# The experts' first products with both halves of the rows in one 512-column matmul, and two changes at the seams

## The reference

```python
# attention: B, H, S, D = 2, 8, 768, 64; a state per head decays by lam
intra = einsum('bhic,bhjc->bhij', qb, kb) * Dmask
out   = einsum('bhij,bhjd->bhid', intra, vb) + (qb * lam_pow) @ kv_state
kv_state = lam_block * kv_state + (kb * rev_pow)^T @ vb

# MLP: 1536 rows, 512 -> 1536 -> 512
x = (silu(x @ w_gate) * (x @ w_val)) @ w_out

# experts: E = 8, F = 1024
expert_idx = argmax(x @ w_gate, axis=1)         # one expert per row
gate_w     = softmax value of the chosen expert
for e in range(E):
    xe = x[expert_idx == e]
    out[expert_idx == e] = gate_w * (maximum(xe @ w1[e], 0.0) @ w2[e])
```

## Time and profile before

| | |
|---|---|
| median of 3 runs | 570.27 us (569.58 to 571.07) |
| profiled execution | 570.9 us, its span 569.3 us |
| busy, share of the span | PE 96%, PEld 82%, DVE 57%, ACT 40%, POOL 14% |
| attention | 0 to 51 us |
| MLP and router | 51 to 361 us |
| index list, first gather | 361 to 374 us |
| experts | 374 to 569 us |

### The profile page before, as it was taken

The page is one execution under the profiler, slowest core; times in us unless marked ns, Lnnn a source line. Parts: engine busy times, 40 slices in busy tenths (PEclk is TensorE's granted clock), DMA queues, the critical chain, the costliest instruction groups (busy, mean ns, idle before and its releaser), DMA issues. The chain is left out here.

```text
span 569.3 us, 8791 instructions
## 1 busy us (share of the span) xinstructions
PE 549.3 (96%) x3290; PEld 468.1 (82%) x3290; DVE 322.4 (57%) x540; ACT 228.9 (40%) x369; POOL 78.6 (14%) x95
## 2 busy tenths in 40 slices
PE   6999999999999999999999999789999999999993
PEld 6888888888878888887888887579999999999982
DVE  8877545444655544545556665446666665766620
ACT  2115323332443432335434553245555554655510
POOL 6972000000000000000000010211130321311101
PEclk9999999999999999999999999979999999999998
DMA  8986433233213243223244545235565757554000
GB/s 295 300 277 209 163 111 107 64 108 111 99 69 122 82 149 111 74 92 111 62 141 151 170 161 221 94 117 209 220 239 181 269 180 246 205 189 164 20 8 34
DMA packets 18432, 84.45 MB, mean 148 GB/s; under 512 B 3036, under 2 KB 3036, under 8 KB 14816
## 3 DMA queue, kind: packets, MB, share of 16 engines
q1 hardware_dynamic: 13536, 71.35, 36.9%
q0 software_dynamic: 3712, 10.54, 5.4%
q10 hardware_dynamic: 1152, 2.13, 1.0%
HBM read 78.73 MB, written 7.39 MB: 151 GB/s over the span
## 5 line engine op out<-in xcount | busy, mean ns | idle before, releaser
L969 DVE TENSOR_TENSOR ewl<-stage,ewh 128x1024 fp32r<-128x1024 f32 x64 | 78.1, 1224 | 23.2 <-ACT ewh L813 23.2
L1090 DVE TENSOR_TENSOR sig<-bank,sig 128x512 f32<-128x512 f32 x36 | 24.9, 692 | 99.0 <-ACT sig L853 99.0
L608 PE MATMUL bank<-xh,gvh 128*128 (+1 forms) x288 | 77.1, 389 | 0.0
L608 PE MATMUL bank<-xl,gvh 128*128 (+1 forms) x288 | 77.0, 389 | 0.0
L608 PE MATMUL bank<-xh,gvl 128*128 (+1 forms) x288 | 77.0, 389 | 0.0
L813 ACT ACTIVATE ewh<-stage 128x1024 fp32r<-128x1024 f32 x64 | 67.0, 1052 | 0.9 <-DMA stage<-expert_w 0.9
L853 ACT ACTIVATE sig<-bank 128x512 f32<-128x512 f32 x36 | 21.7, 602 | 104.4 <-PE bank L608 104.4
L608 PEld LDWEIGHTS bank<-xl,gvh 128*128 128x128 f32 x288 | 54.1, 188 | 11.3
L608 PEld LDWEIGHTS bank<-xh,gvl 128*128 128x128 f32 x288 | 54.1, 188 | 11.2
L608 PEld LDWEIGHTS bank<-xh,gvh 128*128 128x128 f32 x288 | 54.0, 188 | 11.3 <-issue 0.2
L618 PE MATMUL bank<-hh,woh 128*128 128x512 f32 x144 | 56.8, 395 | 0.0
(11 more groups left out here) (144 smaller groups left out, 849.4 us busy)
## 6 DMA issues: line engine op xcount, KB each, us to landing
stage<-expert_w SPq DMA_DIRECT2D x28, 1024.0 KB, 4.9
stage<-mlp_w SPq DMA_DIRECT2D x36, 768.0 KB, 4.4
stage<-attn_in SPq DMA_DIRECT2D x24, 512.0 KB, 5.0
stage<-expert_w POOLq DMA_DIRECT2D x8, 512.0 KB, 5.6
x_rows<-x ACTq DMA_DIRECT2D x8, 260.0 KB, 5.1
x_rows<-x SPq DMA_DIRECT2D x4, 260.0 KB, 4.2
gx<-x_rows,idx POOLq DMA_INDIRECT x16, 4.5
out<-ys,idx POOLq DMA_INDIRECT x16, 3.9
```

The source lines that it names most:

```text
L608: last = mm(bank[:, where, :], wt[:, k, :], (xh, xl)[x][:, k, bass.ds(g * GT, GT)], start=(at == 0), stop=(at == 3 * KD - 1))
L969: V.tensor_tensor(dst, src, high.bitcast(F32), ALU.subtract).then_inc(inc, 1)
L1090: V.tensor_tensor(sig[:, :], bank[:, GATE_BANK, :], sig[:, :], ALU.mult).then_inc(sg_ready, 1)
```

## The change

**First products.** The tiles `exh` and `exl` become one tile `ex` with the high half at z = 0 and the low half at z = 1. `hidden` multiplies the high weights with both halves in one matmul of 512 columns, so that the left half of the PSUM bank gets high by high and the right half high by low; then the low weights with the high rows are added into the left half. The bank's halves have to be added afterwards: ACT copies the right one to `hx` (SBUF), DVE adds the left one to it and writes `hs`, ACT takes the relu of `hs`, and DVE the low half of it. PE's wait for a free bank is now on that addition.

**Rows of the next expert.** Their split and the exponents, all in slot 5 before, are spread over the slots 5, 6 and 7.

**Start.** ACT scales the keys of tile 0 (8 activations of 64 columns), POOL those of the other tiles and not before both decay tables are done; PE does the scores of tile 1 before the first product to the state.

**Before the experts.** POOL reads the number of rounds behind the first two gathers, not ahead of them.

```diff
-        exh = [sb(f"exh{i}", [P, KD, CAP], F32R, region2) for i in range(2)]
-        exl = [sb(f"exl{i}", [P, KD, CAP], F32R, region2) for i in range(2)]
+        ex = [sb(f"ex{i}", [P, 2, KD, CAP], F32R, region2) for i in range(2)]
+        hx = [sb(f"hx{i}", [P, CAP], F32, region2) for i in range(2)]
+        hs = [sb(f"hs{i}", [P, CAP], F32, region2) for i in range(2)]
...
             def keys(n):
                 s = n % 4
                 pool.wait_ge(kv_landed[s], n // 4 * 16 + 16)
-                pool.wait_ge(key_ready, 1)
+                pool.wait_ge(tables_ready, 2)
...
-            for n in range(NT):
+            for n in range(1, NT):
                 if n < LAST_STATE:
                     keys(n)
...
                 gather(0)
                 nc.gpsimd.memset(idx_now[0][:, :], 0).then_inc(now_ready, 2 * E)
                 gather(1)
+                n = read_passes(pool)
...
-            n = read_passes(pool)
-            first_pass()
+            n = first_pass()
...
-                pe.wait_ge(kd_ready, n + 1)
+                if n == 0:
+                    pe.wait_ge(first_keys, H)
+                else:
+                    pe.wait_ge(kd_ready, n)
...
             scores(0)
+            scores(1)
             to_state(0)
-            scores(1)
...
             def hidden(x, par, f):
                 pe.wait_ge(ewl_ready, x * NF2 + f + 1)
                 if f >= 2:
-                    pe.wait_ge(ehl_ready, x * NF2 + f - 1)
-                at = 0
-                for w, z in split_terms:
-                    for k in range(KD):
-                        last = mm(bank[:, H_BANK + f % 2, 0:CAP],
-                                  expert_bufs(par)[w][:, f, k * P:(k + 1) * P], (exh, exl)[z][par][:, k, :],
-                                  start=(at == 0), stop=(at == 3 * KD - 1))
-                        at += 1
+                    pe.wait_ge(hs_ready, x * NF2 + f - 1)
+                where = H_BANK + f % 2
+                for k in range(KD):
+                    mm(bank[:, where, :].rearrange("p (z c) -> p z c", z=2),
+                       expert_bufs(par)[0][:, f, k * P:(k + 1) * P], ex[par][:, :, k, :],
+                       start=(k == 0), stop=False, skip_group_check=True)
+                for k in range(KD):
+                    last = mm(bank[:, where, 0:CAP], expert_bufs(par)[1][:, f, k * P:(k + 1) * P],
+                              ex[par][:, 0, k, :], start=False, stop=(k == KD - 1), skip_group_check=True)
                 last.then_inc(eh_psum, 1)
...
+            act.wait_ge(kv_landed[0], 16)
+            act.wait_ge(key_ready, 1)
+            for h in range(H):
+                nc.scalar.activation(kd[0][:, h, :], att_part(0, 2)[:, h * D:(h + 1) * D], ACT.Copy,
+                                     scale=key_decay[:, h, :]).then_inc(first_keys, 1)
...
             def expert(x, par, more):
                 for f in range(NF2):
                     act.wait_ge(eh_psum, x * NF2 + f + 1)
-                    nc.scalar.activation(ehh[f % 2][:, :], bank[:, H_BANK + f % 2, 0:CAP],
-                                         ACT.Relu).then_inc(ehh_ready, 1)
+                    copy(hx[f % 2][:, :], bank[:, H_BANK + f % 2, CAP:]).then_inc(hx_ready, 1)
+                    act.wait_ge(hs_ready, x * NF2 + f + 1)
+                    nc.scalar.activation(ehh[f % 2][:, :], hs[f % 2][:, :], ACT.Relu).then_inc(ehh_ready, 1)
                     if more:
                         split_expert(1 - par, f, f // 2, expert_loads(x + 1, f // 2))
-                        if f == 5:
-                            tokens(x + 1, 1 - par)
+                        if f >= 5:
+                            (rows_high, rows_high, exponents)[f - 5](x + 1, 1 - par, f - 5)
...
+            def add_terms(x, f):
+                dve.wait_ge(hx_ready, x * NF2 + f + 1)
+                V.tensor_tensor(hs[f % 2][:, :], bank[:, H_BANK + f % 2, 0:CAP], hx[f % 2][:, :],
+                                ALU.add).then_inc(hs_ready, 1)
+
             def expert(x, par, more):
                 for f in range(NF2):
+                    add_terms(x, f)
                     dve.wait_ge(ehh_ready, x * NF2 + f + 1)
-                    V.scalar_tensor_tensor(out=ehl[f % 2][:, :], in0=bank[:, H_BANK + f % 2, 0:CAP], scalar=0.0,
+                    V.scalar_tensor_tensor(out=ehl[f % 2][:, :], in0=hs[f % 2][:, :], scalar=0.0,
                                            in1=ehh[f % 2][:, :].bitcast(F32), op0=ALU.max,
                                            op1=ALU.subtract).then_inc(ehl_ready, 1)
                     if more:
                         split_expert(1 - par, x + 1, f, f // 2)
-                        if f == 5:
-                            tokens(x + 1, 1 - par)
+                        if f >= 5:
+                            (rows_low, rows_low, gates)[f - 5](x + 1, 1 - par, f - 5)
```

More of the change, by code:

```diff
@@ L183, in bass_linear_attention_mlp_moe @@
         qs_ready = sem("qs_ready")
+        first_keys = sem("first_keys")
         kd_ready = sem("kd_ready")
@@ L240, in bass_linear_attention_mlp_moe @@
         eh_psum = sem("eh_psum")
+        hx_ready = sem("hx_ready")
+        hs_ready = sem("hs_ready")
         ehh_ready = sem("ehh_ready")
@@ L472, in first_pass @@
                     scatter(x)
+                return n
             def gather_by_copy(x, par):
@@ L904, in _, with rows_high, exponents @@
                 rows_out(NG - 1, t, t)
[L905 to L909, removed]
+            def rows_high(x, par, i):
+                act.wait_ge(gx_read, x * 2 + i + 3)
+                copy(ex[par][:, 0, :, i * P:(i + 1) * P],
+                     bank[:, T_BANK + i, :].rearrange("p (k i) -> p k i", k=KD)).then_inc(exh_ready, 1)
+            def exponents(x, par, i):
                 act.wait_ge(den_step, x * 2)
@@ L914, in tokens, with first_tokens @@
                 last.then_inc(expo_ready, 1)
+            def first_tokens(x, par):
+                for i in range(2):
+                    rows_high(x, par, i)
+                exponents(x, par, 2)
             def expert(x, par, more):
@@ L933, in last_expert @@
                     act.wait_ge(eh_psum, x * NF2 + f + 1)
-                    nc.scalar.activation(last_hidden(f, 0), bank[:, H_BANK + f % 2, 0:CAP],
-                                         ACT.Relu).then_inc(ehh_ready, 1)
+                    copy(hx[f % 2][:, :], bank[:, H_BANK + f % 2, CAP:]).then_inc(hx_ready, 1)
+                    act.wait_ge(hs_ready, x * NF2 + f + 1)
+                    nc.scalar.activation(last_hidden(f, 0), hs[f % 2][:, :], ACT.Relu).then_inc(ehh_ready, 1)
                 act.wait_ge(y_psum, x * 2 + 1)
@@ L949, in experts @@
                         split_expert(0, f, f // 2, expert_loads(base, f // 2))
-                tokens(base, 0)
+                first_tokens(base, 0)
                 with act.Fori(0, E // 2 - 1) as i:
@@ L1219, in _, with rows_low, gates @@
             V.tensor_scalar(passes[:, :], mosti[:, :], 8, None, ALU.logical_shift_right).then_inc(slots_ready, 1)
-            def tokens(x, par):
-                for i in range(2):
-                    low(exl[par][:, :, i * P:(i + 1) * P], bank[:, T_BANK + i, :].rearrange("p (k i) -> p k i", k=KD),
-                        exh[par][:, :, i * P:(i + 1) * P], exh_ready, x * 2 + i + 1, exl_ready)
+            def rows_low(x, par, i):
+                low(ex[par][:, 1, :, i * P:(i + 1) * P], bank[:, T_BANK + i, :].rearrange("p (k i) -> p k i", k=KD),
+                    ex[par][:, 0, :, i * P:(i + 1) * P], exh_ready, x * 2 + i + 1, exl_ready)
+            def gates(x, par, i):
                 dve.wait_ge(expo_ready, x + 1)
@@ L1230, in tokens, with first_tokens @@
                 V.reciprocal(gate_now[par][:, :], den_eps[:, :]).then_inc(gate_ready_x, 1)
+            def first_tokens(x, par):
+                for i in range(2):
+                    rows_low(x, par, i)
+                gates(x, par, 2)
+            def add_terms(x, f):
+                dve.wait_ge(hx_ready, x * NF2 + f + 1)
+                V.tensor_tensor(hs[f % 2][:, :], bank[:, H_BANK + f % 2, 0:CAP], hx[f % 2][:, :],
+                                ALU.add).then_inc(hs_ready, 1)
             def expert(x, par, more):
                 for f in range(NF2):
+                    add_terms(x, f)
                     dve.wait_ge(ehh_ready, x * NF2 + f + 1)
-                    V.scalar_tensor_tensor(out=ehl[f % 2][:, :], in0=bank[:, H_BANK + f % 2, 0:CAP], scalar=0.0,
+                    V.scalar_tensor_tensor(out=ehl[f % 2][:, :], in0=hs[f % 2][:, :], scalar=0.0,
                                            in1=ehh[f % 2][:, :].bitcast(F32), op0=ALU.max,
@@ L1249, in last_expert @@
                 for f in range(NF2):
+                    add_terms(x, f)
                     dve.wait_ge(ehh_ready, x * NF2 + f + 1)
-                    V.scalar_tensor_tensor(out=last_hidden(f, 1), in0=bank[:, H_BANK + f % 2, 0:CAP], scalar=0.0,
```

(1 more changed line is left out.)

## The result

The changed kernel takes 600.06 us (median of 6 runs, 598.69 to 601.41); the kernel before takes 570.19 beside it (6 runs). Ratio 1.0515, interval 1.0496 to 1.0533: slower by 5%, and 5 us above the 595 forecast. The profiled span went from 569.3 to 598.4 us, +29.1.

What follows compares the result with a forecast made beforehand. It took PE, 96% busy, as the bound before, and DVE as pacemaker after the change. Terms -1.0 - 1.6 + 2.5 + 23.6 + 1.4 = +24.9 on 570.9 gave 595.8; the runs' median is 0.6 lower: 595 us, range 586 to 604.

Steps and rivals of the forecast that it cites:

- Slot of the ring: Mid-expert, DVE and ACT queues: addition, relu, subtraction and weights' split take 2.99 us per slot, against PE's 2.75.
- Addition 0 to addition 7 of an expert: Within one expert on DVE: seven slots of 2.99 plus two row steps of 0.60 us, 22.13 us.
- The overlap of 0.09: In each slot on DVE: back-to-back operations overlap by 0.09 us, taken off the addition's 0.42.
- the hand-over of 0.03: In each slot: passing work between ACT and DVE costs 0.03 us.
- the 0.42 from SBUF: In each slot on ACT: the relu takes 0.42 us reading SBUF, against 0.385 from PSUM.
- PE's way at an expert's end: From the last subtraction to the next expert's first addition: second product, first product and ACT's copy take 3.40 us.
- The clock: Rival: PE's clock falls in the new stalls, about 3 to 4 us in each of 7 experts, 616 to 623; chance 0.08.
- First expert: Expert 0, with the clock low again at its start: 28.2 us against 25.76 before, +2.5.
- Last expert: No weights are split there; 0.6 at its first second product and 0.9 at the drain, less 0.1: +1.4 us.
- First products: On PE: 4 wide and 4 narrow matmuls take 1.376 us, 0.014 less per block, 0.9 us over 64 blocks.
- Start: Kernel start: decay tables at 0.69 us without POOL beside them, -1.0 us; bounds -0.6 and -1.45.
- Seam before the experts: POOL reads the round count after the gather, saving a read of 1.74 us: -1.6 us, bounds -0.8 and -2.3.

Runs made afterwards that it cites:

- ring_open: Changed kernel with DVE's low half of the previous slot's weights moved right behind the addition in slots 1 to 6; 582.87 us, ratio 1.021.
- two_adds: Changed kernel with DVE's addition done twice, first into a tile that nobody reads; 625.07 us, ratio 1.0953.
- relu_on_vector: Changed kernel with the relu on DVE instead of ACT in all experts but the last; 579.39 us, ratio 1.0141.
- wide_no_sum: Changed kernel without ACT's copy and DVE's addition; relu and subtraction read the bank's left half, so the output lacks one product; 568.97 us, ratio 0.9961.
- seams_only: Changed kernel with first products, relu and low half as before (12 narrow matmuls, no copy or addition), both seams kept; 568.06 us, ratio 0.9953.

## Why the prediction was right, and where its terms were off

The direction and the mechanism held; 600.06 lies in the range, 5 above the forecast. Term by term:

- *Slot of the ring.* Predicted 2.99, measured 3.00. Addition 0 to addition 7 of an expert: predicted 22.13, measured 22.16 (458.16 to 480.32). The overlap of 0.09, the hand-over of 0.03 and the 0.42 from SBUF all stand in the rows of the slot. ring_open changes only the order on DVE, two_adds adds one operation to the ring and relu_on_vector takes ACT out of it; the slot becomes 2.76, 3.33 and 2.76. The ring as the limit is shown, not only argued.
- *PE's way at an expert's end.* Predicted 3.40, measured 3.55 (454.61, the end of the subtraction, to 458.16). I took 1.37 for the second product from a stretch without gaps. Behind the wait it is 1.49 from its start to the start of the next product (454.66 to 456.15), because 0.34 us lie between its first two matmuls and 0.23 between the others; the first product behind it takes 1.39, not 1.37. (The 1.66 of the chain counts on to the end of the last matmul, so it is compared only with other rows of the chain.) Per expert that is 27.03 instead of 26.85, 1.1 us in six.
- *The clock.* This is the step that failed, and the largest part of the miss: I priced experts 1 to 6 at full clock, and gave the falling clock a chance of 0.08 as a rival of its own with the price for all seven experts, 3 to 4 us each. A fall cost 1.6 us in the loop, about half of that. It fell behind two of the seven waits, in both profiles of the changed kernel, and cost 2.6 us in experts 1 to 6 (164.8 less 6 x 27.03) and 0.5 in expert 0 (a second product of 2.16 instead of 1.66). My argument against it (0.66 us of work in 2 us and still 1.00) was one row, and the next row of that group already had the fall in it. The Trainium skill, "TensorE: Matmul & The Clock Gate", A second HAM failure mode: psum-queue depth-cycling, which I had set against that row, describes a case of this kind: short idle times between groups of matmuls, with a rate that swings between its two levels. The trace agrees for two waits of seven, and not for the other five, which are as long.
- *First expert.* Predicted 28.2, measured 28.8. The clock was low again at its start, as assumed, and addition 0 came 3.13 after the first matmul (3.36 predicted); the last second product took 2.16, not 1.37.
- *Last expert.* Predicted +1.4, measured +1.8.
- *First products.* I took 0.9 us of PE work as gain where PE is the bound; wide_no_sum shows none. It entered the forecast only through the 1.37 of a block, 1.39 as measured.
- *Start.* Predicted -1.0, measured -0.9 in this profile, with POOL's queries of tile 2 ending the wait, as said. That it came so close is in part luck: three of the eleven profiles show no gain, and I had priced neither a fall of the clock at the start nor late keys.
- *Seam before the experts.* Predicted -1.6 beyond the start's, measured -0.9, near my bound of -0.8. The read of the count was worth up to 1.74, but the gather still came 1.70 behind the count. What it waits for instead, most likely the stored rows' landing, I only argued: the changed kernel's trace does not name it (it shows "issue"), and no run was made to move it. Over the eleven profiles the distance is 1.70 to 2.39 us, so the gain against the one profile of before (2.59) is 0.2 to 0.9.

The rest, -1.0 at the very end, is the landing of the last scatter, which I had not priced: from the end of its issue to the end of the span are 5.5 us in this profile, 5.4 to 5.9 in those of the experiments, seams_only included, and 6.5 in that of before. With it the miss would be 6 us, not 5. All of these profiles have the two seams and there is only one profile of the kernel before, so whether the 1.0 is scatter between executions or comes with the seams stays open; the first products have no part in it, since seams_only has it too. What decides whether a given stall makes the clock fall stays open: the two stalls that did are no longer than the others, though with waits 0.3 us longer (two_adds) it fell behind five of seven.

## What to carry to other kernels

An engine that is busy for two thirds of the time can be the pacemaker: add up, along each in-order queue, the operations and the waits between them from one slot to the same point of the next, and compare that with the bottleneck engine's slot. Before putting a step between two products, look where it stands in the queues; the same work beside the path cost about 3 us here (571.9 against 569.0 without it), in the path it cost 31, and a different order of the same operations gave back 17. Fewer instructions on PE were worth nothing here, since the columns stayed the same.

## What the runs showed of the hardware

- fp32r matmuls here cost by their columns: 4 of 512 take 0.93 us, 12 of 256 take 1.39, 0.116 us per 256 columns either way.
- DVE's product of two SBUF tiles (128x512) takes 1.42 us with POOL's multiplication beside it and 0.69 without.
- DVE's maximum with a constant (128x256, SBUF to fp32r) takes 0.29 us, the two-operand addition and subtraction of that size 0.42.
- Behind a wait of 1.9 us PE's 6 matmuls of 512 columns take 1.49 us from the first start to the next product's, instead of 1.37; 0.34 us lie between the first two starts.
- Behind 4 of 14 such waits (two profiles) the granted clock fell to 0.50 for about 3 us, which cost 1.6 us each in the loop; with 8 matmuls in each wait it fell behind none of 14, and with waits of 2.25 us behind 5 of 7.
